# Two layers and a mixture of experts on one core: a later low part, later column sums, other orders in the first expert pairs and the last

## The reference

```python
def _moe_ref(x, w_in, w_out) -> np.ndarray:
    h = x @ w_in
    g = np.maximum(0.01 * h, h)
    return (g @ w_out).astype(np.float32)

def _moe2_ref(x, w_gate, w1, w2) -> np.ndarray:
    ...
    logits = x @ w_gate
    logits = logits - logits.max()
    P = np.exp(logits)
    for _ in range(8):
        P /= P.sum(1, keepdims=True) + 1e-09
        P /= P.sum(0, keepdims=True) + 1e-09
        P *= N / E
    out = np.zeros((N, D), dtype=np.float32)
    for e in range(E):
        h = np.maximum(x @ w1[e], 0.0)
        ye = h @ w2[e]
        out += P[:, e:e + 1] * ye
    return out.astype(np.float32)
```

## Time and profile before

| what | value |
|---|---|
| time, median of 3 runs (lowest, highest) | 944.05 us (944.04, 945.65) |
| the profiled execution's own time | 943.95 us |
| its span | 942.2 us |
| PE busy, share of the span | 931.0 us, 99% |
| PE weight loads busy | 889.6 us, 94% |
| DVE busy | 645.8 us, 69% |
| POOL busy | 436.2 us, 46% |
| ACT busy | 354.2 us, 38% |
| chain of work that ended last | PE 91%, DVE 6%, ACT 1%, issue 1% |
| granted clock of TensorE | 1.000 |

### The profile page before, as it was taken

How to read it: one execution, slowest core, us unless ns; L and a number is a source line. 1 busy time by engine, 2 the same in 40 slices (tenths; PEclk the granted TensorE clock), 3 DMA queues, 4 the chain that set the end, 5 groups by cost and what they waited for, 6 DMA issues and landing times.

```text
span 942.2 us, 16696 instructions
## 1 busy us (share of the span) xinstructions
PE 931.0 (99%) x6519; PEld 889.6 (94%) x6529; DVE 645.8 (69%) x1066; ACT 354.2 (38%) x671; POOL 436.2 (46%) x489
## 2 busy tenths in 40 slices
PE   8999999999999999999999999999999999999998
PEld 5999888888799999999999999999999999999998
DVE  6787555458778989876666666666667666666664
ACT  5674543353453333333332432333243233323221
POOL 4453131067598655566633652663365266336000
PEclk9999999999999999999999999999999999999999
DMA  7980221011011111111111111111112111110000
GB/s 133 206 145 2 79 77 34 1 35 34 1 34 34 35 35 36 33 46 56 35 34 35 47 55 35 34 35 34 34 44 59 35 35 34 35 34 1 29 29 29
DMA packets 82796, 42.39 MB, mean 45 GB/s; under 512 B 54270, under 2 KB 82302, under 8 KB 82718
## 3 DMA queue, kind: packets, MB, share of 16 engines
q1 hardware_dynamic: 82510, 41.23, 16.9%
q10 hardware_dynamic: 208, 0.11, 0.0%
HBM read 39.13 MB, written 2.11 MB: 44 GB/s over the span
## 4 chain that ended last, share of the span: by engine, by line
PE 91%; DVE 6%; ACT 1%; issue 1%; POOL 0%; DVEq 0%; POOLq 0%; ACTq 0%
PE psB L1657 11%; PE psB L1659 11%; PE psB L1658 11%; PE psA L1643 8%; PE psA L1642 8%; PE psA L1641 8%; PE psA L1640 8%; PE psA L1570 8%; PE psB L1489 2%; PE psA L1468 2%; PE psB L1589 2%; PE psB L1590 2%; PE psB L1591 2%; DVE gl L1393 1%; PE psB L1595 1%
## 5 line engine op out<-in xcount | busy, mean ns | idle before, releaser
L682 POOL TENSOR_TENSOR wst<-raw_w,wst 128x128 fp32r<-128x128 f32 (+2 forms) x192 | 162.9, 861 | 303.9 <-ACT wst L899 175.0
L1657 PE MATMUL psB<-w2s,gh 128*128 128x320 f32 x768 | 238.6, 311 | 0.9 <-DVE acc L1367 0.9
L1659 PE MATMUL psB<-w2s,gl 128*128 128x320 f32 x768 | 237.3, 309 | 0.0
L1658 PE MATMUL psB<-w2s,gh 128*128 128x320 f32 x768 | 237.3, 309 | 0.0
L1393 DVE SCALAR_TENSOR_TENSOR gl<-part,gh 128x512 fp32r<-128x512 f32 x192 | 159.7, 872 | 63.5 <-ACT gh L1014 62.9
L1014 ACT ACTIVATE gh<-part 128x512 fp32r<-128x512 f32 x192 | 110.8, 624 | 244.6 <-DVE part L1387 244.6
L1642 PE MATMUL psA<-xop,wst 128*128 128x256 f32 x672 | 190.2, 283 | 0.0
L1643 PE MATMUL psA<-xop,wst 96*128 96x256 f32 x672 | 190.2, 283 | 0.0
L1641 PE MATMUL psA<-xop,wst 128*128 128x256 f32 x672 | 190.2, 283 | 0.0
L1640 PE MATMUL psA<-xop,wst 128*128 128x256 f32 x672 | 190.0, 283 | 0.0
L1657 PEld LDWEIGHTS psB<-w2s,gh 128*128 128x128 f32 x768 | 144.6, 188 | 1.3 <-DVE gl L1393 1.1
(11 more groups left out here) (194 smaller groups left out, 1377.9 us busy)
## 6 DMA issues: line engine op xcount, KB each, us to landing
raw_w<-in_moe_w_dram SPq DMA_DIRECT2D x32, 320.0 KB, 3.2
raw_w<-in_moe_w_dram SPq DMA_DIRECT2D x32, 256.0 KB, 2.6
raw_w<-in_moe_w_dram SPq DMA_DIRECT2D x96, 64.0 KB, 2.5
qs<-in_q_dram SPq DMA_DIRECT2D x12, 160.0 KB, 3.5
ks<-in_k_dram SPq DMA_DIRECT2D x12, 160.0 KB, 3.8
vz<-in_v_dram SPq DMA_DIRECT2D x12, 160.0 KB, 3.6
og<-in_o_gate_dram SPq DMA_DIRECT2D x12, 160.0 KB, 3.7
out_dram<-acc SPq DMA_DIRECT2D x5, 320.0 KB, 2.4
```

Of the source, the lines that this page charges most:

```text
L682: return pool.tensor_tensor(dst, raw, high.bitcast(F32), ALU.subtract)
L1657: pe.matmul(bank, gh[:, slot, cols], w2[:, f, 0, :], start=first, stop=False)
L1658: pe.matmul(bank, gh[:, slot, cols], w2[:, f, 1, :], start=False, stop=False)
L1659: last = pe.matmul(bank, gl[:, slot, cols], w2[:, f, 0, :], start=False, stop=end)
```

## The change

1. `mlp_block` of DVE: `leaky_low` is now that of the tile before, and stands behind the leaky step of this tile; one last `leaky_low` comes behind the whole part. At the third tile of a block the first `read_y` stands ahead of the leaky step. `leak` waits in addition for `g_ready`, that is, until the low part of two tiles ago, which stands just ahead of it in the queue, is done (it overwrites what that reads).
2. ACT: the cast `pair_s_high(HALVES, 1)` leaves the last block of the two-layer part and comes first in `middle(0)`, behind the copy of product 1 of pair 0.
3. DVE, pair 4: the four `read_o` stand between `low_of(4, 1)` and `low_of(4, 0)`. At later blocks they stay behind both.
4. DVE, rounds: `read_columns` stands behind `low_of(n, 1)`, and PE's `column_sums` behind `behind(n, 1)`.
5. PE, end: `behind(96, k)` is one row quarter of both feature tiles in place of two quarters of one tile; it waits for both low parts at once.

```diff
@@ ACT, mlp_block and middle
                         if (tb, f) == (2, 7):
                             pair_w2_high(HALVES, 1)
-                            pair_s_high(HALVES, 1)
...
                 s, at = HALVES + n // BP, n % BP
+                if n == 0:
+                    pair_s_high(s, 1)
                 if at == 0:
                     pair_w1_high(s, 3)
@@ DVE
             def leak(u, f):
                 dve.wait_ge(hs_ok, u + 1)
+                dve.wait_ge(g_ready, RING + u - 1)
...
                     u = (half * NTB + tb) * NF + f
-                    leak(u, f)
-                    read = half + tb > 0 and f == LAG - 1
                     before = (half, tb - 1) if tb else (half - 1, NTB - 1)
-                    if read:
+                    if half + tb > 0 and f == LAG - 1:
                         read_y(*before, 0)
-                    leaky_low(u, f)
-                    if read:
+                        leak(u, f)
                         for t in range(1, KT + 1):
                             read_y(*before, t)
+                    else:
+                        leak(u, f)
+                    leaky_low(u - 1, (f - 1) % NF)
...
             low_parts(NU // U_IT, -1)
-            leaky_low(1, 1)
...
                 mlp_block(1, tb)
+            leaky_low(HALVES * NTB * NF - 1, NF - 1)
...
+            def read_block(blk):
+
+                if blk < NTB:
+                    dve.wait_ge(xl, XL * (blk + 1))
+                for j in range(JT):
+                    read_o(blk - 1, j)
+
             def pair(n):
 
                 blk, p = n // PP, n % PP
                 add_up(n)
+                low_of(n, 1)
+                if n == PP:
+                    read_block(blk)
                 if n - 1 in ROUND_AT:
                     read_columns(ROUND_AT.index(n - 1))
-                low_of(n, 1)
                 low_of(n, 0)
...
-                if p == 0 and n > 0:
-                    if blk < NTB:
-                        dve.wait_ge(xl, XL * (blk + 1))
-                    for j in range(JT):
-                        read_o(blk - 1, j)
+                if p == 0 and n > PP:
+                    read_block(blk)
@@ PE, behind and pair
+                if n == NP:
+                    if k == 0:
+                        pe.wait_ge(g2, 2 * m + 2)
+                    for f in (1, 0):
+                        expert_out(m, f, (k,))
+                    return
...
                     pe.wait_ge(p1_read, n + 1)
+                behind(n, 1)
                 if n - 1 in ROUND_AT:
                     column_sums(ROUND_AT.index(n - 1))
-                behind(n, 1)
```

## The result

The changed kernel is slower: 948.31 us median of 7 executions (946.80 to 949.99) against 944.05; ratio 1.0039, interval 1.0026 to 1.0051. The forecast was 944.7, range 941.9 to 946.5. The profiled execution took 948.31, its span is 946.6. One of the seven executions of the kernel before that were taken beside it took 3250.64 us; nothing on record explains it, and no comparison here rests on it.

What follows compares the result with a forecast made beforehand. TensorE was taken as the bound, with VectorE just under it as second. Terms -1.70 - 0.65 + 3.1 + 0 = +0.75 on the profiled execution's 943.95 us gave 944.7 us, range 941.9 to 946.5.

Steps and rivals of the forecast that it cites:

- if a quarter falls away ... I take the middle, +3.1: Rounds: a quarter of some 8 us of VectorE waiting on GpSimd may vanish, +2.2; middle with +4.0 is +3.1 us.
- 1  leaky order: Two-layer part: finished-block sums no longer late for TensorE at two tile boundaries, -1.70 us; ends 0 and -1.70.
- 2,3 A(6) beside part 1: VectorE's first add of expert pair 6: 0 to 1.3 us earlier beside the leaky order's shift; middle -0.65 us.
- 4  rounds: Column sums and their later reading in the expert rounds: +3.1 us, between +2.2 and +4.0.
- 5  last pair: Last pair's output order: load about 0.1 us late, last addition about 0.1 sooner; taken 0, ends -0.1 and +0.1.
- Part 2: Moved weight cast: 0 by itself; with the leaky order, two x sums lose 0.24 us each, 0.5 off VectorE's chain.
- between 0 and 0.8 us may come off: Pair 4: the second low part, moved behind the acc copies, may get 0 to 0.8 us shorter.
- 0.4 us more than by the middle: Pair 4: second low part waits for GpSimd's instruction to end, saving nothing; sum 0.4 us above the middle.
- I take 0.65 us a round: Rounds: the reading leaves VectorE's pause and stands between the low parts, costing 0.65 us in each of six rounds.
- P(15) = A(14) + 4.44: TensorE's third product of pair 15 starts 4.44 us after VectorE's first add of pair 14, waiting for the reduce.
- DVE's queue in the rounds costs it all: Rival, third products of pairs 7, 9, 13, 15: +4.0 us with nothing earlier at pair 6, 946.3 us; chance 0.17.
- marks given for the profile: Signs of being right, including no acc wait at pair 5 and 70.5 us from pair 6's first add to pair 16's third product.

Runs made afterwards that it cites:

- e3: Kernel before with only the leaky order of the two-layer part (low part behind the next tile's leaky step): 942.13 us in executions without a clock fall.
- e6: Changed kernel with the rounds' edit undone on both engines, all other parts kept: 941.5 us without a clock fall, median 942.54.
- e4: Kernel before with only the rounds' edit, on both TensorE and VectorE: 950.67 us, 949.20 in its one execution without a clock fall.
- e5: Kernel before with only the last pair's new order: 943.40 us without a clock fall.
- d2: Changed kernel with GpSimd's 128x512 low part of the weight sums issued as two of 128x256: 945.6 us without a clock fall.
- e2: Changed kernel with TensorE's column sums put back ahead of the second stretch of expert outputs, VectorE's reading still late: 946.8 us.
- h4: Kernel before with nothing changed but GpSimd's long operations cut into pieces: 942.7 us without a clock fall.
- d1: Changed kernel with VectorE's reading of the column sums one step later still, behind both low parts of the pair: 949.58 us.
- e7: Changed kernel with the column sums read early in pair 12 alone: 949.03 us, 947.69 without a clock fall.
- e1: Changed kernel with VectorE's column-sum reading put back ahead of the first low part, TensorE's sums still late: 942.42 us without a clock fall.
- d3: Changed kernel without the rounds' edit on either engine, GpSimd's 128x512 low part issued as two of 128x256: 941.38 us.

## Why the prediction was wrong

The step that failed is the one in part 4 on the meetings, "if a quarter falls away ... I take the middle, +3.1": the rounds cost 5.3 us, since the meetings grew where they had been taken to shrink. Part 3's 0.65 us did not come either (0.1), and a fall of the clock, 1.5 us, had no term. By the prediction's own terms, at full clock:

```
term                               forecast   measured   from
1  leaky order                     -1.70      -1.8       e3
2,3 A(6) beside part 1             -0.65      -0.1       e6 against e3
4  rounds                          +3.1       +5.3       e4 (5.25); changed against e6
5  last pair                        0         -0.5       e5
sum                                +0.75      +2.9
a fall of the clock                 -         +1.5       in four of seven executions, twice in one
```

Where the fall lies is known for the profiled execution alone (behind pair 13).

**Part 1** was right in mechanism and size: no sum is late, and nothing behind gave it back.

**Part 2** was to give up to 0.5 us (half of it is in the -0.65), by shorter x sums, and gave nothing that can be seen. In the changed kernel the first of them still takes 0.92 us (at 289.87). The second takes 0.69 instead of 1.12, but so it does in e3, which doesn't move the cast. The moved cast brings A(0) forward by 0.9 us (267.73 in e3, 266.83 in e6), and by A(4) nothing of it is left (300.60 and 300.64).

**Part 3** failed at the step "between 0 and 0.8 us may come off": A(5) - A(4) fell by 0.11, from 8.19 (e3) to 8.08 (e6). The reading of the 3.23 us was off too: the two low parts before are 1.24 and 2.07 us, so the first was done at 307.1, not 307.5, and 1.4 of the 1.94 us belonged to the second. DVE's and POOL's timelines of the changed kernel, against the earlier trace rows:

```profile
305.23 1.67 DVE L1369 COPY acc<-psB 128x320 f32<-128x320 f32 x4
306.82 1.73 DVE L1395 SCALAR_TENSOR_TENSOR gl<-part,gh 128x512 fp32r<-128x512 f32 x1
...
306.71 2.99 POOL L682 TENSOR_TENSOR wst<-raw_w,wst 128x512 fp32r<-128x512 f32 x2
```

The copies end, and the second low part is issued 0.11 us behind a POOL instruction of 1.29 us and ends 0.55 us after it. It takes 1.73 us, against 2.07 in the old order and 0.64 where nothing meets it, so it is held nearly as long as before. The prediction had written this case down, by the Trainium skill's rule (page "SBUF — State Buffer", section "Who interferes with whom"), "0.4 us more than by the middle", and then took the middle; the row had already shown the rule at work, and its value should have been the term. d2, in which that POOL instruction is halved, got 0.55 us at this place and 0.27 by A(6).

**Part 4** held the mechanism and missed the size. Its steps one by one:
- "I take 0.65 us a round": measured 0.57. A(7) - A(6) rose by 0.57, A(8) - A(7) by 0.57. Six of them make 3.4, not 3.9. This step was good.
- "if a quarter falls away ... I take the middle, +3.1": this is the step that failed. The new order did not deal the meetings in DVE's favour but against it, by about 1.5 us (61.04 in e2, less 56.15 and 3.4). Summed by kind between A(6) and A(14), e2 against before, the six normalisings by columns took 1.9 us more (two at 1.35, one at 1.62), the column readings' small instructions 0.6 more, the row normings 0.8 less and the low parts 0.65 less; with 4.2 us of pauses, and 0.45 less by closer starts, that makes the 4.9. By this count the pauses cost 3.7 and the meetings 1.2. I had bounded the meetings on one side only, from zero down to a quarter less; the rows gave no reason for a sign. With +1.5 instead of -0.9 the same sum gives +4.0 - 0.5 + 1.5 = 5.0, and 0.3 remain, which lie between A(14) and P(16) (11.78 in e2, 11.54 in the forecast).
- "P(15) = A(14) + 4.44": the path ended earlier. Nothing waits at pair 15; the last wait is at pair 13, P(13) = A(12) + 4.88, 0.4 over the forecast's distance because pair 12's first low part takes 1.23 us. From there PE goes at its own pace (21.17 us to P(16) in e2).
- No term for the clock. The forecast had the wait ("1 to 1.5 us at the first"), but not that a fall of the clock would follow the longest, 1.5 us. This is the part of the median that neither the pauses nor the meetings explain.

The rival "DVE's queue in the rounds costs it all" named the right mechanism. Its price, 946.3, is 0.5 under the time at full clock; its places were nearly right (waits at pairs 7, 9, 12 and 13, forecast 7, 9, 13 and 15). But it stood at an end of the range with a chance of 0.17, and it is the case that came.

**Part 5** was taken as 0 with ends of 0.1. DVE's last read ends no earlier relative to PE. The gain is in the stores, which I had not looked at: three leave at 942.61, 943.49 and 944.37, formerly at 938.58, 939.04 and 939.51, and those of 160 KB land 1.8 us behind their issue, not 2.3 (median of two).

Of the marks given for the profile, these came: no wait for ysum, tiles every 3.62 us, new waits for the reduce with 1.13 us at the first, 1.22 us between the low parts. The wait for acc, which was to go, is 0.2. P(16) - A(6) came out at 74.35, or 72.8 at full clock, where 70.5 was given.

## What to carry to other kernels

An instruction that stands in the pause of its engine is free there and costs its time anywhere else (0.57 us a round here); before it is moved, look at what the engine would do in that pause instead. Where two engines hold each other up for whole instructions, as VectorE and GpSimd do here, any shift of one of them deals the meetings anew, so a term for them needs both signs; and it can be made small by cutting the long instructions of the engine that has time (here POOL, 46% busy), which brought 1.2 us by itself (h4), turned the late sums and the early reading of pair 12 from a loss into a gain, and still left the late reading a loss of 4.0. A wait is a symptom: if it can be moved without moving the end (e2), look for the queue behind it.

## What the runs showed of the hardware

- The clock falls seen in profiles, with what PE did before them: idle 1.66 us (changed kernel and e4), 1.73 and 1.88 (d1), 2.37 (e7); each was followed, 0.3 us (e4) to 1.5 us (d1, the second) after PE went on, by 3.4 us at the 1.2 GHz level, and cost 1.5 us or a little more. Behind the idle stretches of 1.0 to 1.14 us at pairs 7, 9, 12 and 13 none is seen in any trace, nor behind e1's of 1.27 and d3's of 1.43. The counts go the same way: changed, e4, d1 and e7 have a fall in 15 of 20 executions; e2 and d2, the same order of the rounds on DVE with no such wait above 1.14 us, in 3 of 15.
- Another fall belongs to no edit. In e5's profile it lies at 20 to 30 us (in those of h4 and d1 too), and A(0) is 1.6 us later than in before's:

```profile
20.00:30.00 10.00, 9.29 (x67) 8.57 (x66) 5.71 (x17) 5.45 (x11) 3.74 (x6) 0.83 0.90 206
```

  It, or one like it, is in some executions of every kernel that had ten or more (five of ten of e6, four of ten of e3), before included (4 of the 25 beside e5 and e6 were about 1.6 us longer); what brings it on in one execution and not in the next stays open.
- A DVE instruction of 96 or fewer elements a partition can take 1.35 to 1.62 us instead of 0.17 to 0.25 beside a POOL instruction. The reduces of the same table (L1330, L1344) took 0.24 to 0.26 us in every trace.
- The two last stores of 160 KB landed 1.8 us (median) behind their issue where the stores are issued 0.88 us apart (changed, e5), and 2.3 us where they are 0.47 apart (before). That the spacing is the cause is not shown.
